# Attention and two MLPs on one core: normalising after PV, by reciprocals spread through DRAM, and PV in longer runs

## What is computed

```python
mask = q_assign[:, :, :, None] == k_assign[:, :, None, :]     # 16 clusters, nearest centroid of q and of k
scores = np.where(mask, scale * np.matmul(q, k.transpose(0, 1, 3, 2)), -1e9)
attn = np.exp(scores - np.max(scores, axis=-1, keepdims=True))
attn = attn / (np.sum(attn, axis=-1, keepdims=True) + 1e-09)
x = np.matmul(attn, v)                                        # 2 x 8 heads, 768 tokens, 64 wide
x = x.transpose(0, 2, 1, 3).reshape(B * S, H * D)             # 1536 x 512
h = (x @ w1) * (x @ w2) @ w3 @ w_out                          # 512 -> 1024 -> 1024 -> 512
h = h @ w_in                                                  # 512 -> 2048
out = (h * np.clip(h + 3.0, 0.0, 6.0) / 6.0) @ w_out2         # 2048 -> 512
```

## Time and profile before

| | before |
|---|---|
| median of the runs | 741.24 us |
| the profiled execution | 740.81 us |
| its span, first to last instruction | 738.8 us |
| TensorE busy | 719.2 us (97%) |
| VectorE busy | 483.0 us (65%) |
| ScalarE busy | 418.0 us (57%) |
| GpSimd busy | 511.1 us (69%) |
| granted TensorE clock, mean | 1.000 |

### The profile page before, as it was taken

The page is one execution under the profiler, slowest core; times in us unless marked ns, Lnnn a source line. Parts: engine busy times, 40 slices in busy tenths (PEclk is TensorE's granted clock), DMA queues, the critical chain, the costliest instruction groups (busy, mean ns, idle before and its releaser), DMA issues.

```text
span 738.8 us, 11957 instructions
## 1 busy us (share of the span) xinstructions
PE 719.2 (97%) x4001; PEld 595.6 (81%) x4001; DVE 483.0 (65%) x865; ACT 418.0 (57%) x855; POOL 511.1 (69%) x534
## 2 busy tenths in 40 slices
PE   6998999999999999999999999999999999999998
PEld 5776666666666665899999999999988879998886
DVE  5327666776677777567886778878865436885221
ACT  6225766676667677445445454477754446775333
POOL 4957776767766778897796987968647748762321
PEclk9999999999999999999999999999999999999999
DMA  9655634636447300222001120011211223221212
GB/s 320 155 152 148 165 91 116 152 85 171 93 112 177 69 29 0 86 72 73 1 29 56 60 86 1 29 55 67 81 58 58 72 99 115 72 72 58 71 43 85
DMA packets 34571, 65.29 MB, mean 88 GB/s; under 512 B 5328, under 2 KB 10448, under 8 KB 34512
## 3 DMA queue, kind: packets, MB, share of 16 engines
q1 hardware_dynamic: 32928, 61.66, 28.6%
q10 hardware_dynamic: 1584, 2.88, 1.0%
HBM read 40.93 MB, written 3.15 MB: 60 GB/s over the span
## 4 chain that ended last, share of the span: by engine, by line
PE 84%; POOL 5%; DVE 4%; ACT 2%; DMA 2%; SPq 2%; issue 1%; ACTq 0%; POOLq 0%
PE ps L1219 18%; PE ps L1221 18%; PE ps L1220 18%; PE ps L1323 10%; PE ps L1309 8%; PE ps L1297 6%; PE ps L1299 4%; DVE g_lo L1135 1%; POOL b_lo L504 1%; DVE sum_lo L1101 1%; PE ps L1267 1%; DMA wo_raw<-in_wo 1%; PE ps L1284 1%; DMA stage<-in_w 1%; POOL probs L545 1%
## 5 line engine op out<-in xcount | busy, mean ns | idle before, releaser
L579 POOL TENSOR_TENSOR b_lo<-stage,b_hi 128x512 fp32r<-128x512 f32 x94 | 111.5, 1187 | 112.8 <-ACT b_hi L792 110.9
L545 POOL TENSOR_SCALAR probs<-probs,recips 128x768 f32<-128x768 f32 x96 | 87.4, 911 | 61.1 <-DVE recips L1041 61.0
L1035 DVE TENSOR_REDUCE neg_max<-ps 128x1 f32<-128x768 f32 x96 | 91.4, 953 | 55.0 <-PE ps L1299 54.8
L1135 DVE TENSOR_TENSOR g_lo<-gate,g_hi 128x384 fp32r<-128x384 f32 x96 | 79.9, 840 | 68.9 <-ACT g_hi L858 68.8
L730 ACT ACTIVATE probs<-ps,neg_max 128x768 f32<-128x768 f32 x96 | 86.6, 902 | 17.3 <-DVE neg_max L1035 14.7
L858 ACT CAST g_hi<-gate 128x384 fp32r<-128x384 f32 x96 | 48.8, 514 | 83.7 <-PE ps L1221 83.6
L1323 PE MATMUL ps<-probs_t,v_raw 128*64 128x384 f32 x384 | 82.0, 510 | 0.0
L1309 PE MATMUL ps<-ident,probs 128*128 128x128 f32 x576 | 78.8, 272 | 1.1 <-POOL probs L545 1.0
L1219 PE MATMUL ps<-b_hi,g_hi 128*128 128x512 f32 x192 | 75.0, 390 | 2.0 <-DVE g_lo L1135 2.0
L806 ACT COPY probs_t<-ps 128x512 f32<-128x512 f32 x96 | 56.0, 583 | 35.3 <-PE ps L1309 33.8
L1221 PE MATMUL ps<-b_hi,g_lo 128*128 128x512 f32 x192 | 74.8, 389 | 0.0
(11 more groups left out here) (118 smaller groups left out, 1852.9 us busy)
## 6 DMA issues: line engine op xcount, KB each, us to landing
stage<-in_wio SPq DMA_DIRECT2D x64, 256.0 KB, 2.5
stage<-in_w SPq DMA_DIRECT2D x48, 256.0 KB, 3.0
qk_ops<-qk_split SPq DMA_DIRECT2D x32, 384.0 KB, 4.9
qk_raw<-in_qk SPq DMA_DIRECT2D x16, 384.0 KB, 5.3
qk_ops<-qk_split SPq DMA_DIRECT2D x32, 192.0 KB, 4.8
v_raw<-in_v SPq DMA_DIRECT2D x16, 192.0 KB, 2.6
out<-out_sb ACTq DMA_DIRECT2D x11, 256.0 KB, 2.1
wo_raw<-in_wo SPq DMA_DIRECT2D x8, 256.0 KB, 5.7
```

Of the source, the lines that this page charges most:

```text
L545: nc.gpsimd.tensor_scalar(probs[s % PROBS][:], probs[s % PROBS][:], recips[:, s:s + 1], 1.0, ALU.mult, ALU.mult).then_inc(s_norm, 1)
L579: nc.gpsimd.tensor_tensor(b_lo[n % 2][:, cols], stage[n % 2][:, cols], b_hi[n % 2][:, cols].bitcast(F32), ALU.subtract).then_inc(s_lo[half ...
L1035: nc.vector.tensor_reduce(neg_max[:, g:g + 1], scores[g % 2], AX.X, ALU.max, negate=True).then_inc(s_max, 1)
L1135: nc.vector.tensor_tensor(g_lo[i][:], hidden(q, c, f)[0][:], g_hi[i][:].bitcast(F32), ALU.subtract).then_inc(s_glo, 1)
```

## The change

The exponentials are transposed and multiplied by V as they are. Once per unit VectorE makes all six columns of reciprocals (`reciprocals`); SP stores them to DRAM, waits for that, and loads them back, spread over the 64 partitions of each head's output (`spread_recips`), into the place that x_hi will take. VectorE multiplies PV's result by them into x_raw (`x_normed`), which lies where x_lo will be. ScalarE rounds from there, and x_low is GpSimd's, but for the last unit. PV runs as step 0 ahead of the score of slot 2 of a unit, step 1 behind its transposes, steps 2 and 3 in slot 4, steps 4 and 5 in the next slot 0. VectorE copies groups 0, 2 and 7, in some slots ahead of the maxima. The logit rows are copied one slot later, the mask rows ahead of x_high, q is scaled one slot later. The sums of the first wide block move into slots 86 to 95. Functions that only moved are left out below.

```diff
@@ -31,10 +31,11 @@
-DVE_GROUPS = (2, 5, 8)
+DVE_GROUPS = (0, 2, 7)
+PV_STEPS = {0: (4, 5), 2: (1,), 4: (2, 3)}
@@ -229,6 +230,7 @@
+        recip_all, x_raw = sb("recip_all", [P, KT * TOK], at=base), sb("x_raw", [P, KT * TOK], at=base + 4 * KT * TOK)
@@ -300,6 +302,7 @@
+        recip_rows = nc.dram_tensor("recip_rows", (2, 2 * HALF), F32, kind="Internal").ap()
@@ -318,9 +321,9 @@
-        s_recip, s_norm = sem("recip_ready"), sem("probs_normalised")
+        s_recip, s_rrow, s_rall = sem("recips_ready"), sem("recip_rows_in"), [sem(f"recips_spread{i}") for i in range(2)]
-        s_xh, s_xl = sem("x_hi_ready"), sem("x_lo_ready")
+        s_xr, s_xh, s_xl = sem("x_ready"), sem("x_hi_ready"), sem("x_lo_ready")
@@ -480,6 +483,16 @@
+            def spread_recips(u):
+                sp.wait_ge(s_recip, u + 1)
+                rows = recip_rows[u % 2]
+                sp.dma_start(rows.rearrange("(k p t) -> p k t", k=2, t=3),
+                             recips[:, u * ST:(u + 1) * ST].rearrange("p (k t) -> p k t", k=2)).then_inc(s_rrow, 16)
+                sp.wait_ge(s_rrow, 16 * (u + 1))
+                for k in range(2):
+                    sp.dma_start(recip_all[k * D:(k + 1) * D, x_cols(u)], rows[k * HALF:(k + 1) * HALF].partition_broadcast(D)
+                                 ).then_inc(s_rall[u % 2], 16)
             for n in range(2, HEADS):
@@ -488,6 +501,10 @@
+                if n >= 3:
+                    spread_recips(n - 3)
+            for u in range(UNITS - 3, UNITS):
+                spread_recips(u)
@@ -540,10 +557,10 @@
-            def normalise(s):
-                pool.wait_ge(s_recip, s + 1)
-                nc.gpsimd.tensor_scalar(probs[s % PROBS][:], probs[s % PROBS][:], recips[:, s:s + 1], 1.0,
-                                        ALU.mult, ALU.mult).then_inc(s_norm, 1)
+            def x_low(unit):
+                pool.wait_ge(s_xh, unit + 1)
+                nc.gpsimd.tensor_tensor(x_lo[:, x_cols(unit)], x_raw[:, x_cols(unit)],
+                                        x_hi[:, x_cols(unit)].bitcast(F32), ALU.subtract).then_inc(s_xl, 1)
@@ -657,21 +674,24 @@
-            for s in range(SLOTS):
-                normalise(s)
-                mix_parts(0, "attention", s)
+            for s in range(SLOTS + 1):
+                if s < SLOTS:
+                    mix_parts(0, "attention", s)
+                if s == SLOTS - 10:
+                    weight_sums(GATE0)
+                    last_weight_sum(GATE0)
+                if s % ST == 0 and s >= 2 * ST:
+                    x_low(s // ST - 2)
-                    if step == 0:
+                    if step == 1:
-                    if step == 1:
+                    if step == 2:
-                    if step in (2, 3):
-                        split_lo(n, step - 2)
+                        split_lo(n, 0)
+                        split_lo(n, 1)
-            weight_sums(GATE0)
-            last_weight_sum(GATE0)
@@ -731,8 +751,8 @@
             def x_high(unit):
-                act.wait_ge(s_pv, unit + 1)
-                nc.scalar.copy(x_hi[:, x_cols(unit)], ps[:, PV_BANKS[unit % 2], 0:HALF]).then_inc(s_xh, 1)
+                act.wait_ge(s_xr, unit + 1)
+                nc.scalar.copy(x_hi[:, x_cols(unit)], x_raw[:, x_cols(unit)]).then_inc(s_xh, 1)
@@ -767,6 +787,16 @@
+            def sums_high(n, last):
...
             def mix_high(q, part, step):
@@ -792,10 +822,13 @@
             for s in range(SLOTS + 1):
+                n, step = prepared(s)
                 if s + 1 < SLOTS:
                     exp(s + 1)
+                if n is not None and step == 2:
+                    rows_of_logits(n)
-                    unit, i = divmod(s - 1, ST)
+                    unit = (s - 1) // ST
@@ -805,26 +838,17 @@
-                    if i == ST - 1 and unit >= 1:
-                        x_high(unit - 1)
-                n, step = prepared(s)
-                if n is not None and step == 1:
-                    rows_of_logits(n)
+                mix_high(0, "attention", s)
+                if s == SLOTS - 6:
+                    sums_high(GATE0, False)
+                if s == SLOTS - 5:
+                    sums_high(GATE0, True)
+                if s == SLOTS - 2:
+                    block_high_next(GATE0 + 1, 0)
                     mask_rows(n)
-                mix_high(0, "attention", s)
-                if s == SLOTS - 2:
-                    block_high_next(GATE0 + 1, 0)
-            def sums_high(n, last):
...
+                if s % ST == 0 and s >= 2 * ST:
+                    x_high(s // ST - 2)
@@ -881,8 +905,6 @@
-            sums_high(GATE0, False)
-            sums_high(GATE0, True)
@@ -898,8 +920,6 @@
-                    if g == 0:
-                        x_high(UNITS - 1)
@@ -917,6 +937,8 @@
+                    if g == 0:
+                        x_high(UNITS - 1)
@@ -1034,16 +1056,32 @@
-            def reciprocal(s):
-                dve.wait_ge(s_exp, s + 1)
-                step(nc.vector.tensor_scalar(sums1[:, s:s + 1], sums[:, s:s + 1], 1e-9, None, ALU.add))
+            def reciprocals(u):
+                cols = slice(u * ST, (u + 1) * ST)
+                dve.wait_ge(s_exp, (u + 1) * ST)
+                step(nc.vector.tensor_scalar(sums1[:, cols], sums[:, cols], 1e-9, None, ALU.add))
-                nc.vector.reciprocal(recips[:, s:s + 1], sums1[:, s:s + 1]).then_inc(s_recip, 1)
-            def x_low(unit):
-                dve.wait_ge(s_xh, unit + 1)
-                nc.vector.tensor_tensor(x_lo[:, x_cols(unit)], ps[:, PV_BANKS[unit % 2], 0:HALF],
-                                        x_hi[:, x_cols(unit)].bitcast(F32), ALU.subtract).then_inc(s_xl, 1)
+                nc.vector.reciprocal(recips[:, cols], sums1[:, cols]).then_inc(s_recip, 1)
+            def x_normed(unit):
+                dve.wait_ge(s_pv, unit + 1)
+                dve.wait_ge(s_rall[unit % 2], 32 * (unit // 2 + 1))
+                cols = x_cols(unit)
+                nc.vector.tensor_tensor(x_raw[:, cols].rearrange("p (t q) -> p t q", t=3),
+                                        ps[:, PV_BANKS[unit % 2], 0:HALF].rearrange("p (t q) -> p t q", t=3),
+                                        recip_all[:, cols].rearrange("p (q t) -> p t q", t=3), ALU.mult).then_inc(s_xr, 1)
+            def sums_low(n, last):
...
+            def last_x_low():
+                dve.wait_ge(s_xh, UNITS)
+                cols = x_cols(UNITS - 1)
+                nc.vector.tensor_tensor(x_lo[:, cols], x_raw[:, cols], x_hi[:, cols].bitcast(F32), ALU.subtract).then_inc(s_xl, 1)
@@ -1067,39 +1105,42 @@
+            def group_copies(s):
+                unit = (s - 1) // ST
+                for k in groups_of(s - 1):
+                    if k % GROUPS in DVE_GROUPS:
+                        use = ("probs", k)
+                        if unit >= 2:
+                            dve.wait_ge(s_pv, unit - 1)
+                        dve.wait_ge(s_fill[ring_bank(use)], ring_turn(use) + 1)
+                        at = k % GROUPS * GROUP
+                        nc.vector.tensor_copy(probs_t[:, unit % 2, at:at + GROUP, :].rearrange("p a b -> p (a b)"), ring(use)
+                                              ).then_inc(s_rel[ring_bank(use)], 1)
             for s in range(SLOTS + 1):
-                if s < SLOTS:
-                    reciprocal(s)
+                groups_first = s % ST in (0, 4, 5)
+                if s >= 1 and groups_first:
+                    group_copies(s)
                 if s + 2 < SLOTS:
                     row_max(s + 2)
-                if s >= 1:
-                    unit, i = divmod(s - 1, ST)
-                    for k in groups_of(s - 1):
-                        if k % GROUPS in DVE_GROUPS:
-                            use = ("probs", k)
-                            if unit >= 2:
-                                dve.wait_ge(s_pv, unit - 1)
-                            dve.wait_ge(s_fill[ring_bank(use)], ring_turn(use) + 1)
-                            at = k % GROUPS * GROUP
-                            nc.vector.tensor_copy(probs_t[:, unit % 2, at:at + GROUP, :].rearrange("p a b -> p (a b)"), ring(use)
-                                                  ).then_inc(s_rel[ring_bank(use)], 1)
-                    if i == ST - 1 and unit >= 1:
-                        x_low(unit - 1)
-                if n is not None and step_of == 3:
-                    best_of(n)
+                if s >= 1 and not groups_first:
+                    group_copies(s)
+                if s % ST == 0 and s >= ST:
+                    reciprocals(s // ST - 1)
+                if s % ST == 0 and s >= 2 * ST:
+                    x_normed(s // ST - 2)
-            def sums_low(n, last):
...
+                if s == SLOTS - 2:
+                    sums_low(GATE0, False)
+                if s == SLOTS - 1:
+                    sums_low(GATE0, True)
+                if n is not None and step_of == 3:
+                    best_of(n)
@@ -1142,8 +1183,6 @@
```

(35 more changed lines are left out.)

13 lines of the change are left out of this document (5 added, 8 removed).

## The result

| | before | changed |
|---|---|---|
| median | 741.59 us (741.0 to 744.52, 20 runs) | **745.15 us** (740.21 to 749.57, 20 runs) |
| ratio | | 1.0042 [1.0024, 1.0061] |
| the profiled execution, its span | 740.81, 738.8 us | 747.12, 745.1 us |
| TensorE busy | 719.2 us | 713.6 us |
| GpSimd busy | 511.1 us | 444.3 us |

The account below looks back on a forecast made before the run. TensorE was taken as the bound, fully busy from 75 to 282 us. 740.81 - 9.9 + 2.9 - 1.0 - 1.3 = 731.5, forecast as 732 us; range 727.5 to 737, extended to 742 to hold 8 in 10.

Parts of the forecast that it names:

- The PV term: TensorE, units 0 to 14: two joined PV steps per unit save 0.33 us each, 9.9 us less in all.
- the Trainium skill's rule on spacing: TensorE: spacing goes by columns, so joined steps save nothing; as a rival 742 us, chance 0.03.
- The hand-over term: Each unit's end: PV, x_normed, x_high, exponential; TensorE stalls 0.2 us in 14 units, 2.9 us more.
- The ends: First and last attention slots: less work on the other engines saves 1.3 us in the first, 1.0 in the last.
- I take 2.5 ... Thin, but hidden: SP's queue: store lands in 2.5 us; an odd head's spread needs 16.7 of 16.9 us, so costs nothing.
- SP's part of a spread, put at nothing: SP's store, wait and two broadcasts per unit: hidden while SP keeps up with TensorE's 29.1 us pair, no cost.
- L: Landing time of the reciprocals' store: SP needs 23.2 + 2L per pair, keeping up to 2.95; expected reading 2.1 to 2.9.
- the odd head: Spread behind an odd head's loads: 16.9 us from the releasing score to x_normed, SP needs 16.7; hidden.
- The rival of SP's wait: SP's queue: the store's landing becomes the bound, 747 us at 4.0, outweighing the gain from 3.6 on; chance 0.15.
- The weight sums: First wide block's sums, moved into slots 86 to 95: nothing gained, cost nothing, at most 0.5 us.

Follow-up runs that it names:

- early-store version: The changed kernel with SP issuing the reciprocals' store ahead of the mask rows, waiting and broadcasting behind them, ahead of the v loads: 731.26 us, again 731.22.
- 24-byte pieces: The changed kernel with the reciprocals' store cut into 128 pieces of 24 B instead of 256 of 12 B: 735.68 us.
- odd heads alone: The changed kernel with the reciprocals' store ahead of the mask rows and the broadcasts ahead of the v loads for odd heads only: 732.24 us.

## Why the prediction was wrong

**The PV term, right.** 9.9 us from 30 joined steps: the period of 14.30 in the early-store version, a PV run of 1.44 and score pairs of 0.35 in the changed kernel. From the score of slot 10 (75.77 before, 75.58 with the early store) to the last unit's PV block (296.98 and 286.25), 10.5 us are saved: 9.9 and the tail. By the Trainium skill's rule on spacing ("TensorE: Matmul & The Clock Gate", Back-to-back issue gap), which it gives for an isolated matmul, the order of kinds would have been worth nothing; the trace disagrees in both kernels (0.55 and 0.36 before, 0.55 and 0.35 in the changed one).

**The hand-over term, 2.9 too much.** In the early-store version it is 0. TensorE's side was right: 4.19 from slot 5's score to PV's end (4.2), 2.5 from there to the score that needs the exponential. VectorE's side was taken as a sum of durations, 4.6 to 4.7, and is 4.20: in the timeline operations of 0.95, 0.69 and 0.95 follow each other at 0.93, 0.61 and 0.86, each beginning a little before the end of the last. x_raw starts 0.05 behind PV, not 0.5.

**The ends, 1.1 to 1.5 too much.** First slots 0.2 instead of 1.3, counted from the span's start. That start is no firm mark: in versions with the same code up to there, slot 10's score stands at 75.03 to 78.20. Counted from the product with the hot columns at 60.94 and 61.36, it is 0.6. In either case less than taken: there the chain is the preparation of the masks (best, hot, hot_cols), which the change leaves alone. Tail 0.6 instead of 1.0. Together with the term above these errors cancel in part. So it is luck that the early-store version, at 731.3, came out so near the sum.

**The step that failed: "I take 2.5 ... Thin, but hidden".** It has three faults, and SP's part of a spread, put at nothing, was worth some 14 us.
First, the size of L. The store landed in 3.1 at the median and 5.9 at most; I took it from transfers of other shapes and named 2.9 as the upper end of what would be seen. Second, the odd head. It had 16.9 us by my count and needed 16.7. In the case shown it had 16.4 (from the release of the loads at 131.60 to PV's end at 148.0; VectorE was not late, so its 0.5 was no reserve), and it needed 18.8, until the broadcasts landed at 150.44: 11.3 of issues, 2.8, 0.5, and 4.1 for a broadcast that I had at 2.6 and that is in flight beside the next head's copies (that these slow it was not tried). So here the broadcast has 1.5 of the 2.1 us by which the need was mis-sized, and the store 0.3; the stalls up to 184.84 and 247.00 stand behind stores of 4.5 and 5.9. Third, a margin of 0.2 us was judged as if landings had one value. Where two nearly equal chains meet in each unit, every long landing is a stall and no short one pays it back. And the sum had no term for the clock: behind the idle times of 2.16 and 3.46 us it fell, some 3.3 us more, behind that of 2.00 it did not.

**The rival of SP's wait, right in mechanism and place, off in its point.** It was to outweigh the gain from L = 3.6 on. It did at a median of 3.1. Its formula gives 23.2 + 2 x 3.1 = 29.4 for a pair, and 29.9 at the mean of the twelve landings from 83.40 on, 3.35. The six pairs of the trace, from the store of an odd head to the next, take 29.24 to 32.95, 30.85 on average (83.40 to 268.48). So SP's own work comes close to the 30.0 of the kernel before, and about 1 us of each pair is neither issue nor landing. SP stood idle for TensorE five times, for 8.7 us, while TensorE stood idle for SP for 11.8. Throughput at a mean landing alone would have left the changed kernel no slower than before; what it leaves out is that each side waits for the other, head by head. That is read from the chain of waits and from both idle times. The runs with 24-byte pieces and with odd heads alone fit it, but they would fit a full queue as well, as both take SP's need below TensorE's 28.6. Its chance of 0.15 was too low for a step whose margin was 0.2 and whose main term no row showed.
The Trainium skill's rule beside it ("DMA: Bandwidth & Descriptors", Specifications) is that transfers under 512 B do a read-modify-write. The runs don't bear it out as the cause: 128 pieces of 24 B landed in 1.6 and 128 of 512 B in 1.5. Twice as many pieces, of half the size, took 1.0 longer.

**The weight sums, right against before, not in the change.** Moving them gains nothing over the kernel before, as it had no gap there. But in the changed kernel's order they would have cost 1.9 in the old place, by the chain because x_low now stands ahead of them. I looked at the edit alone and not at what another edit puts ahead of it.

What stays open: why landings of one and the same store reach from 2.2 to 5.9 us, why one stall of 2 us was followed by a lower clock and another was not, and how the 13.9 us divide between the store's move and that of the broadcasts.

## What to carry to other kernels

Price a wait inside a DMA queue by the latency of its whole loop, head by head, against its longest landing, and not only by the throughput of the queue at a mean landing. If the margin is thinner than the spread of the landings, issue the transfer earlier and wait for it behind other issues. Before two edits are costed one by one, ask which slack hid each of them and whether the other takes it: here the PV runs brought 3.4 us alone, and in the early-store version undoing them cost 14.6, of which 9.9 was their own price and the rest the hand-over that single steps meet. Join the pieces of a small store where you can: one piece a partition instead of two was worth 9.5 us.

## What the runs showed of the hardware

A 3 KB store landed in 2.6 us in 256 pieces of 12 B and in 1.6 in 128 pieces of 24 B; 128 pieces of 512 B took 1.5. The landing of the same store varied by 3.7 us within one execution (2.2 to 5.9). TensorE's granted clock was 0.56 in the 3.7 us behind an idle time of 2.16 us, after being 1.00 before; behind an idle time of 2.00 us in the same execution it stayed at 1.00. And operations of VectorE that follow each other overlapped at their ends by 0.02 to 0.09 us, so that the sum of their mean durations, 4.6 to 4.7, came out above the chain's 4.20.
